# Spectral mixing and two feed-forward layers on one core: other slots for side work, another order for the last pair

## The reference, cut to what matters

```python
X = np.fft.rfft(x, axis=1)                 # x: 2 x 3008 x 256
y = np.fft.irfft(X * (filt_r + 1j*filt_i), n=3008, axis=1)
x = y.reshape(6016, 256)
h = x @ w_in                               # 256 -> 2048
g = np.maximum(h, 0.0) + alpha * np.minimum(h, 0.0)
x = g @ w_out                              # 2048 -> 256
h = np.maximum(x @ w2_in, 0.0)
out = h * h @ w2_out
```

## Time and profile before

| what | value |
|---|---|
| median of 3 runs | 1115.47 us (1115.47 to 1116.11) |
| the profiled execution's own time | 1114.61 us |
| its span in the trace | 1112.8 us |
| PE busy | 1104.5 us, 99% |
| DVE busy | 961.5 us, 86% |
| ACT busy | 663.0 us |
| POOL busy | 650.6 us |
| granted TensorE clock | full in all 40 slices |

### The profile page before, as it was taken

How to read it: one execution, slowest core, us unless ns; L and a number is a source line. 1 busy time by engine, 2 the same in 40 slices (tenths; PEclk the granted TensorE clock), 3 DMA queues, 4 the chain that set the end, 5 groups by cost and what they waited for, 6 DMA issues and landing times.

```text
span 1112.8 us, 17230 instructions
## 1 busy us (share of the span) xinstructions
PE 1104.5 (99%) x6911; PEld 985.2 (89%) x6911; DVE 961.5 (86%) x1099; ACT 663.0 (60%) x785; POOL 650.6 (58%) x479
## 2 busy tenths in 40 slices
...
DMA packets 57752, 88.28 MB, mean 79 GB/s; under 512 B 4808, under 2 KB 45384, under 8 KB 57672
## 3 DMA queue, kind: packets, MB, share of 16 engines
...
q10 hardware_dynamic: 200, 0.15, 0.0%
...
## 4 chain that ended last, share of the span: by engine, by line
PE 92%; DVE 4%; POOL 1%; DMA 1%; ACT 1%; issue 1%; SPq 0%; DVEq 0%; ACTq 0%; POOLq 0%
PE bank L1140 15%; PE bank L1145 15%; PE bank L1141 15%; PE bank L1179 13%; PE bank L1168 13%; PE bank L1166 13%; PE bank L1117 2%; DVE g_lo L915 1%; PE bank L987 1%; PE bank L1042 1%; PE bank L1040 1%; DVE g_raw L930 1%; PE bank L1019 1%; PE bank L1000 0%; PE bank L1050 0%
## 5 line engine op out<-in xcount | busy, mean ns | idle before, releaser
L614 POOL TENSOR_TENSOR g_raw<-g_raw 128x250 f32<-128x250 f32 (+1 forms) x191 | 281.0, 1471 | 391.1 <-DVE g_raw L940 391.1
L915 DVE TENSOR_TENSOR g_lo<-g_raw,g_hi 128x1750 fp32r<-128x1750 f32 (+1 forms) x191 | 424.2, 2221 | 45.1 <-ACT g_hi L626 44.5
L750 ACT ACTIVATE g_raw<-bank 128x500 f32<-128x500 f32 (+1 forms) x384 | 226.4, 591 | 320.4 <-PE bank L1145 281.1
L626 ACT ACTIVATE g_hi<-g_raw 128x1750 fp32r<-128x1750 f32 (+1 forms) x191 | 318.9, 1670 | 50.7 <-POOL g_raw L617 49.3
L1168 PE MATMUL bank<-g_hi,w_lo 128*128 128x250 f32 (+1 forms) x1337 | 320.1, 279 | 0.0
L1166 PE MATMUL bank<-g_hi,w_hi 128*128 128x250 f32 (+1 forms) x1337 | 319.5, 279 | 0.0
L1140 PE MATMUL bank<-in_hi,w_hi 128*128 128x500 f32 (+1 forms) x768 | 302.2, 394 | 2.0 <-DVE g_raw L930 2.0
L1141 PE MATMUL bank<-in_hi,w_lo 128*128 128x500 f32 (+1 forms) x768 | 298.3, 388 | 0.0
L1168 PEld LDWEIGHTS bank<-g_hi,w_lo 128*128 128x128 f32 x1337 | 252.7, 189 | 7.5
L1166 PEld LDWEIGHTS bank<-g_hi,w_hi 128*128 128x128 f32 x1337 | 252.5, 189 | 7.4
L617 POOL TENSOR_TENSOR g_raw<-g_raw 128x250 f32<-128x250 f32 (+1 forms) x191 | 247.8, 1298 | 15.0
...
## 6 DMA issues: line engine op xcount, KB each, us to landing
filt_b<-filt SPq DMA_DIRECT2D x36, 256.0 KB, 4.7
v_rows<-v_out_b SPq DMA_DIRECT2D x24, 256.0 KB, 4.0
vc<-v_rows SPq DMA_DIRECT2D x22, 256.0 KB
...
```

What stands on the lines that cost most here:

```text
L614: pool.tensor_tensor(g_raw[:, r, T2, 0:h], g_raw[:, r, B22, 0:h], g_raw[:, r, T1N, 0:h], ALU.add).then_inc(t2_ready, 1)
L626: return act.activation(dst, src, ACT.Copy)
L750: act.activation(g_raw[:, r, 2 * j:2 * j + 2, 0:h], h_ps[j][:, 0:2 * h].rearrange("p (j d) -> p j d", j=2), ACT.Relu, scale=-1.0 if n < SL ...
L915: dve.tensor_tensor(g_lo[:, q, B11:T4 + 1, 0:h], g_raw[:, q, B11:T4 + 1, 0:h], g_hi[:, q, :, 0:h], ALU.subtract).then_inc(g_lo_ready, 1)
```

## The change

1. Spectra: `B_SLOT` becomes 11, 12, 14, 15, 19, 20, 22, 23, 27, 28, 30, 31. The low part of the loaded rows stands in POOL's slot b-1 or, from the third unit on, in slot b itself where b % 8 is 3 or 4. The buffers for the products go from 2 to 3 (`deep`).
2. Weights of the second layer: `W2_SLOT` becomes 38, 45, 51, 58, 66, 74, 82, 88.
3. POOL: in a slot the low parts stand ahead of `add`.
4. The last pair: another order of slot 190's and 191's products. Product (3, 0) of the last group sums in a bank of its own (`y_ps[0]`), and the last operation of `combine` is two, one for either product of bank 3.
5. Constants: the small transform's matrix gets a tensor and a DMA of its own, the unread matrix is dropped, and `const_full` moves to memory that is reused later.

```diff
-F_A1, F_X = 0, ROWS
-F_V, F_W, F_I = F_X + P, F_X + 2 * P, F_X + 3 * P
+F_V, F_W, F_I = 0, P, 2 * P
...
-B_SLOT = [12, 14, 16, 20, 22, 24, 28, 30, 32, 34, 36, 38]
+B_SLOT = [11, 12, 14, 15, 19, 20, 22, 23, 27, 28, 30, 31]
+
+T_LOW = [slot if u > 1 and slot % FP in (3, 4) else slot - 1 for u, slot in enumerate(B_SLOT)]
...
-W2_SLOT = [45, 51, 57, 63, 69, 75, 81, 88]
+W2_SLOT = [38, 45, 51, 58, 66, 74, 82, 88]
...
-        const_full = sb(ctx, "const_full", [P, FULL_COLS])
+        const_a1_sb = sb(ctx, "const_a1", [ROWS, ROWS])
...
+        const_full = sb(before, "const_full", [P, FULL_COLS])
...
-        f1 = Spectral(f1_scope, ctx, nc, "b1", 1, deep=2, raw=2, ...
+        f1 = Spectral(f1_scope, ctx, nc, "b1", 1, deep=3, raw=2, ...
...
             load_w1(0)
+            sp.dma_start(const_a1_sb[:, :], consts_full[0:ROWS, FULL_COLS:FULL_COLS + ROWS]).then_inc(const_a1_loaded, 16)
...
                 if n < SLOTS_1:
                     for u in range(B_UNITS):
-                        if B_SLOT[u] + 1 == n:
-                            add(u)
-                    for u in range(B_UNITS):
-                        if B_SLOT[u] - 1 == n:
+                        if T_LOW[u] == n:
                             pool.wait_ge(f1.t_hi_ready, u + 1)
                             low(f1.t_lo[:, u % f1.raw, :], ...
...
+                    for u in range(B_UNITS):
+                        if B_SLOT[u] + 1 == n:
+                            add(u)
...
-            act.wait_ge(c_ready, 4 * LAST_G + 4)
+            act.wait_ge(c_ready, 4 * LAST_G + 5)
...
+                if g == LAST_G:
+
+                    dve.wait_ge(m3_done, 1)
+                    dve.tensor_tensor(ct[:, C12, 0:h], y_ps[0][:, 0:h], ct[:, U4, 0:h], ALU.add).then_inc(c_ready, 1)
+                    dve.wait_ge(down_done, (g + 1) * FP)
+                    dve.tensor_tensor(ct[:, C21, 0:h], m_ps[3][:, 256:256 + h], ct[:, U3, 0:h],
+                                      ALU.add).then_inc(c_ready, 1)
+                    return
...
+            def sum_at(g, b, side):
+
+                if g == LAST_G and (b, side) == (3, 0):
+                    return y_ps[0][:, 0:LAST_H]
+                return m_ps[b][:, side * 256:side * 256 + HALF[g % GROUPS]]
...
-                    if last and (b, side) in ((0, 0), (1, 1), (2, 1)) or final and b == 0:
+                    if (last or final) and (b, side) in ((0, 0), (1, 1), (2, 1)):
                         mm.then_inc(m_done, 1)
...
-            down_high(LAST_N - 1)
             pe.wait_ge(s_sums_ready, FP)
+
+
+            down_high(LAST_N - 1, PRODUCTS[:5])
             pe.wait_ge(g_ready, 2 * LAST_N + 2)
-
-            down_last(PRODUCTS[:2])
+            down_last(PRODUCTS[:4])
             down_low(LAST_N - 1, PRODUCTS[:3])
-            down_last(PRODUCTS[2:3])
+            down_last(PRODUCTS[4:5])
             down_low(LAST_N - 1, PRODUCTS[3:5])
-            down_last(PRODUCTS[3:5])
-            down_low(LAST_N - 1, PRODUCTS[5:])
-            down_last(PRODUCTS[5:])
+            for product in (PRODUCTS[5:6], PRODUCTS[6:]):
+                down_high(LAST_N - 1, product)
+                down_low(LAST_N - 1, product)
+                down_last(product)
```

More of the change, by code:

```diff
@@ L260, in spectral_mix_two_ffn @@
         f1_scope = ExitStack()
-        f1 = Spectral(f1_scope, ctx, nc, "b1", 1, deep=2, raw=2, filters=2, v_raw=2, x_raw=4, a_raw=4, group=1,
+        f1 = Spectral(f1_scope, ctx, nc, "b1", 1, deep=3, raw=2, filters=2, v_raw=2, x_raw=4, a_raw=4, group=1,
                       a_ps=bank[6:8], x_ps=bank[6:7], v_ps=bank[7:8])
@@ L601, in _ @@
                                 f1.y_lo_ready)
-                    for q in range(FP):
-                        for at, a, b in W2_LOW:
-                            if W2_SLOT[q] + at == n:
-                                pool.wait_ge(s_hi_ready, q + 1)
-                                low(s_lo[:, a:b, :], s_raw[:, a:b, :], s_hi[:, a:b, :], s_lo_ready)
+                    for u in range(B_UNITS):
+                        if B_SLOT[u] + 1 == n:
+                            add(u)
+                for q in range(FP):
+                    for at, a, b in W2_LOW:
+                        if W2_SLOT[q] + at == n:
+                            pool.wait_ge(s_hi_ready, q + 1)
+                            low(s_lo[:, a:b, :], s_raw[:, a:b, :], s_hi[:, a:b, :], s_lo_ready)
                 if LATE_W <= n + 2 < FP:
@@ L1018, in transform_1 @@
                 pe.wait_ge(f1.x_loaded[u % f1.xs], (u - AHEAD_A) // f1.xs * 16 + 16)
-                pe.matmul(f1.a_ps[ps][0:ROWS, :], const_full[0:ROWS, F_A1:F_A1 + ROWS], f1.x_raw[:, u % f1.xs, :],
+                pe.matmul(f1.a_ps[ps][0:ROWS, :], const_a1_sb[:, :], f1.x_raw[:, u % f1.xs, :],
                           start=True, stop=True).then_inc(f1.a_done, 1)
@@ L1156, in down_high @@
                 pe.wait_ge(g_hi_ready, n + 1)
-                for b, side, tile, piece in PRODUCTS:
-                    o = m_ps[b][:, side * 256:side * 256 + h]
+                for b, side, tile, piece in products:
+                    o = sum_at(g, b, side)
                     if first and g > 0 and side == 0:
```

32 lines of the change are left out of this document (15 added, 17 removed).

## The result

The changed kernel is slower: 1119.43 us (median of 7 runs, 1118.60 to 1121.36) against 1115.72 for the kernel before beside it (1115.10 to 1116.89), ratio 1.0035 with a 95% interval of 1.0023 to 1.0046. The forecast was 1112.2 with a range up to 1115.2: the sign is wrong and the time lies outside the range.

A forecast was written before the change was run, and what follows sets the result against it. PE's own work plus its waits bounds the kernel, and only waits can be won. Terms -1.41 - 1.78 + 0.20 - 0.26 = -3.25 us took 1115.47 to 1112.2, range 1110.9 to 1115.2.

The forecast's parts named there:

- Part 1, slot 35: Slot 35's wait of 1.30 us and the restart of 0.11 behind it go: -1.41 us.
- No pair should stall: 0: Slots behind two spectra in a row: no PE stall, 0 us, covered by 1.4 us to spare.
- lateness: Time from a slot's start to DVE's first L930 or L933; forecast 3.64 us after a pair's first unit.
- Part 3: Slots 13, 21, 29: a third POOL operation ahead of T2, priced at 1.5 us, covered, so 0.
- POOL holds DVE off: Rival: POOL's low parts in a row block L915 or products by up to 1.5 us; 1113.5 us, chance 0.10.
- The pairs stall PE: Rival: second spectra wait in slots 12, 15, 20, 23, 28, 31; 8.5 us in all, 1120.7 us, chance 0.07.
- either sign by which the forecast was to be wrong: `up` waits for L930 above 0.5 us before slot 90, or PE waiting before a spectrum.
- Part 2, the sums: Moved block sums: waits behind slots 58, 82, 64 go, -1.78 us; sums in 59, 67, 75, 83 add 0.20.
- the rival of 2.08: Rival: sums cost 2.08 us with p = 3 too, 1.13 each in four slots; 1116.5 us; chance 0.15, fully or partly.
- Part 2, slot 39 at 0: Sums moved into slot 39 cost PE nothing: 5.13 us against the slot's 5.15.
- Part 4: Kernel's end: DVE's last addition finishes at 1109.92 instead of 1110.18, -0.26 us; bounds 0 and -0.6.
- Part 5: Constants: one more small DMA among early loads, hidden by PE's first 60 us: 0; bounds -0.2 to +0.2.

The follow-up runs named there:

- e1: The changed kernel with GpSimd's old order: addition ahead of the low parts, each loaded rows' low part a slot before its unit; 1114.14 us, ratio 0.9981.
- e6: e1 with TensorE's y matmuls and next spectrum waiting for the real products (`re_ready`) instead of the imaginary ones; 1114.36 us, ratio 0.9985.
- e13: The kernel before with the unit of slot 34 in slot 35, block sums in other new slots, and the change's new end and constants; 1113.69 us, ratio 0.9982.
- e4: The changed kernel with the block sums back in the slots of the kernel before; 1120.18 us, ratio 1.0036.

## Why the prediction was wrong

**Part 1, slot 35: right.** 7.30 went to 6.68 with an inverse of 0.70 now in it, slot 36 to 5.16: the 1.41 came.

**Part 1, "No pair should stall: 0": wrong.** The working followed two things behind a pair: when `up` may write its banks, and when a spectrum finds its own. It passed over slot p = 5 as one "which PE fills with `y_group` for over 7 us", as if that were cover. But `y_group` itself waits for the products of the pair's second unit. That wait had 1.3 us to spare in the kernel before, and it had no term. The lateness too came out higher: 4.65 into slot 12 for 3.64, and 6.89 into slot 13 for 4.16 (4.82 in e1). Into slot 15, behind the second pair's first unit, it was the 3.64 that was said, but only since PE's wait in slot 13 had let DVE catch up: in e1, without that wait, it is 6.01. e1 and e6 show that even with GpSimd's old order, the best that ran with pairs, these slots take 193.8 - 191.4 = 2.4 us too long, more than the 1.41 that the pairs remove.

**Part 3, the step that failed.** The third operation on POOL was priced at 1.5 us, put "wholly on the chain T2, T4, g_hi, g_lo", found to be covered there, and counted as 0. Its real victim was the instruction of DVE beside it, four products in a row, which lost 1.0 us to each low part (dose table). The removal of `add`'s 1.27 us of waiting was taken as free. With two low parts and T4 beside the products, the y matmuls made their slots 2.1 to 2.2 us longer three times, 6.3 us, and a clock drop of 1.7 us followed the first: 8.0 where the sum had 0.

**The rival "POOL holds DVE off" had the mechanism, not the place.** It named low parts in a row that block L915 or the products, and let "the pairs' spare 1.4" hide nearly all of it: 1113.5. The Trainium skill, "SBUF — State Buffer", section "SBUF: two separate sides", has the two engines exclude each other for a whole instruction; the trace agrees here (a product of 0.34 took 1.38 and ended 0.14 behind a POOL instruction of 1.34). What was missing was to count the instructions on both sides: four short ones of DVE beside three of POOL's (0.79, 1.34, 1.31) waited three times and not once, and took 3.66 for 1.13. The range fell short because this rival was priced at its least.

**The rival "The pairs stall PE" came nearest in number, by luck.** It gave 1120.7 for the 1119.43 measured. But its six places, slots 12, 15, 20, 23, 28 and 31, show no excess over 0.1 us (5.84, 6.52, 5.84, 6.55, 5.91, 6.60), and its mechanism, a spectrum that waits, did not occur in the change. Nor did either sign by which the forecast was to be wrong; only the list of slot lengths from 12 to 36 showed the fault, in slots 13, 21 and 29.

**Part 2, the sums: right.** VectorE at the end of slot 59, kernel after:

```profile
420.74 0.28 DVE L843 SCALAR_TENSOR_TENSOR s_raw<-s_raw 128x128 f32<-128x128 f32 x1
...
421.79 1.37 DVE L942 SCALAR_TENSOR_TENSOR g_raw<-g_raw,rest_sb,bank 128x500 f32<-128x500 f32 x2
```

421.79 - 420.74 = 1.05, the cheap price (1.06), with POOL idle since 418.99; the rival of 2.08 fell. Slots 60, 68 and 84 are at 5.15, so the 0.20 that was added is nothing. Slots 58 to 95 won 1.82 (said: 1.78 less the 0.20). Slot 91's excess stayed, as said, and e13 shows that it goes with the sums of slot 89.

**Part 2, slot 39 at 0: off by 0.23.** Slot 39 itself took 5.16, as said, but the lateness was worked out for the slot of the sums alone. The same series has a low part in slot 41, p = 1, and there DVE's block differences ran beside it. VectorE, kernel after, then GpSimd:

```profile
318.63 1.74 DVE L952 TENSOR_TENSOR g_raw<-g_raw 128x500 f32<-128x500 f32 x1
```

```profile
318.53 1.30 POOL L555 TENSOR_TENSOR s_lo<-s_raw,s_hi 128x512 fp32r<-128x512 f32 x1
```

1.74 for 0.68 put `combine` and the next L942 about a microsecond back, and slot 43 took 6.21 for 5.98. e4, without that series, has 5.97.

**Part 4: right**, 0.36 for the 0.26 that was said; the additions followed each other as worked out (the working had 1107.37 + 0.71 as 1108.11, which is 0.03 too much). **Part 5: right**: slots 0 to 10 take 60.92 and 60.93.

**The sum.** Said: -3.25. By the slots: -1.41 - 1.82 + 0.23 - 0.36 = -3.4 for the parts that were counted, and +8.0 for the wait that wasn't: +4.6, against 4.8 of the spans, in which slot 0 also began 0.3 later. The medians differ by 3.7, since the profiled execution of the kernel before lay 1.1 below the median of the runs beside the change.
